# Moving the sum of the two half banks of an attention head from VectorE to ScalarE copies, transfers and GpSimd

## The chip, the cores and the metric

One core of a Trainium2 chip runs the whole kernel. The metric is the device time of one launch in microseconds (us). Engines are called by their names in the profile: PE is TensorE (PEld its weight loads), ACT is ScalarE, DVE is VectorE, POOL is GpSimd, SP is SyncE, which issues nearly all transfers.

## What is computed

A clustered attention (2 batches, 8 heads, 768 tokens, head width 64, 16 clusters per head) feeds two dense layers on 1536 tokens. Attention sees only pairs of tokens in the same cluster. The cut reference:

```python
mask = q_assign[:, :, :, None] == k_assign[:, :, None, :]
scores = scale * np.matmul(q, k.transpose(0, 1, 3, 2))
scores = np.where(mask, scores, -1000000000.0)
attn = np.exp(scores - np.max(scores, axis=-1, keepdims=True))
attn = attn / (np.sum(attn, axis=-1, keepdims=True) + 1e-09)
x = np.matmul(attn, v)                     # (B, H, S, D)
x = x.transpose(0, 2, 1, 3).reshape(B * S, H * D)
# then: h = x @ w_in; g = h * sigmoid(1.702 h); x = g @ w_out
# then: h = x @ w_in2; softmax-gated, normalised, times gains; out = ... @ w_out2
```

Matrices are split into a high part in the matmul's reduced format and a low part (the value less its high part), and products of parts are summed, so that the result keeps the accuracy of f32.

## The kernel before

**Stages.** The attention takes the first 250 us or so, the first dense layer (48 turns of weights) comes next, the second one is last.

**The attention loop.** It has 8 iterations `it` (a pair of heads, j = 0 and 1, in each) of 12 steps `n`; a step is a tile of 128 query rows, so a head has 6 steps and a half head 3. Each engine runs its own list of the same steps with lags, in the order in which the code issues them; a wait on a semaphore holds up everything behind it on its engine. In a step:

- PE: `turn` transposes the normalised rows of step n-6 (L534), then come parts of `head_half` (12 matmuls of 384 columns for a half head, spread over three steps, L551), `scores_of` (L515, L519) and, in iterations 0 to 5, one of four small pieces of the next clusters ("lots": `sims_of`, `tokens_of`, `ties_of`, `first_of` in steps 1, 4, 7, 10).
- ACT: in steps 2, 5, 8 and 11 first `x_of_low_v` (L784); then `turned_high` (two casts, L778), `exps` (L767), in steps 5 and 11 `kq_high` (L736), in steps 7 and 10 `x_high` (L790), and in steps 1 and 7 a copy for the lots (L719, L727).
- DVE: `row_max` (L958), row sums and their `inverse` (L966, L972, once for a pair of steps, two steps later), `turned_low` (two subtractions, L978), in one step of three `x_sum` (L986), and the lots' `compare` and `choose`.
- POOL: `probs` times the inverse (L1237), splits of q, k and v for the next iteration, and `x_low` (L1196) in steps 8 and 11. Its step n comes when the inverse of its pair is there, so it runs some two steps behind the others. A tiny instruction, `carry_waits` (L1161), stands ahead of several of them and takes their wait.
- SP: loads, and `place_head`, which moves parts between partitions.

**The half head's sum.** v is laid out as high beside low, so the 128 rows of a half head's bank hold the product with the high part of v in 64 rows and with the low part in the other 64; for the second head of the pair the halves are swapped. The two must be added. ACT copies the low rows of the bank to their place in `x_sums`, and DVE adds the high rows out of the bank to it:

```python
nc.scalar.copy(x_flat[D * j:D * j + D, bass.ds(x_tokens(it, n), HALF)],
               head_out(half)[D * (1 - j):D * (1 - j) + D, :]).then_inc(x_low_v_done, 1)
nc.vector.tensor_tensor(x_flat[rows, at], head_out(half)[rows, :], x_flat[rows, at], ALU.add
                        ).then_inc(x_done, 1)
```

The bank is free for PE when `x_done` has counted. With both heads of a pair summed, ACT's `x_high` casts 128 rows to `xh` and POOL's `x_low` makes `xl`, which the first dense layer reads.

Of the kernel before, what the change touches and what calls it, by code (L numbers as in the profile page):

```python
# [12 lines left out]
P = 128  # L13
# [3 lines left out]
def clustered_attention_two_mlps(nc, q_t, k_t, v_r, cent, w_gelu, w_ln, gains, out):  # L17
# [29 lines left out]
    with ExitStack() as ctx:  # L47
# [50 lines left out]
        upl = [sb(f"upl{u}", [P, DM], F32R) for u in range(2)]  # L98
        downh = [sb(f"downh{u}", [P, DM], F32R) for u in range(2)]
# [16 lines left out]
        row_inv = sb("row_inv", [P, NP], F32, early)  # L116
        probs_th = [sb(f"probs_th{h}", [P, QT, HALF], F32R, early) for h in range(2)]
# [91 lines left out]
        x_low_v_done = sem("x_low_v_done")  # L209
        x_done = sem("x_done")  # L210
# [70 lines left out]
        X_STEPS = [(c * CH + QT + CH - 1 + X_LAG + 1) % STEPS for c in range(2)]  # L281
# [5 lines left out]
        def x_tokens(it, n):  # L287

            return (it % HP) * T + (it // HP) * S + (n % QT) // CH * HALF
# [15 lines left out]
        def _(sp):  # L305
# [78 lines left out]
            for it in range(1, ITS):  # L384
# [9 lines left out]
                load_ln(it)  # L394

# [44 lines left out]
        def _(pe):  # L440
# [7 lines left out]
            def sims_of(e):  # L448
# [4 lines left out]
                if e > LOT_LEAD:  # L453
                    pe.wait_ge(x_done, (e - LOT_LEAD) * 4 - 3)
# [7 lines left out]
            def tokens_of(e):  # L462
# [3 lines left out]
                if e > LOT_LEAD:  # L466
                    pe.wait_ge(x_done, (e - LOT_LEAD) * 4 - 2)
# [6 lines left out]
            def ties_of(e):  # L474
                pe.wait_ge(compared, e + 1)
                if e > LOT_LEAD:
                    pe.wait_ge(x_done, (e - LOT_LEAD) * 4 - 1)
# [6 lines left out]
            def first_of(e):  # L484
# [3 lines left out]
                if e > LOT_LEAD:  # L488
                    pe.wait_ge(x_done, (e - LOT_LEAD) * 4)
# [223 lines left out]
        def _(act):  # L713
# [66 lines left out]

            def x_of_low_v(it, n):
                j, half = n // QT, n // CH
                act.wait_ge(head_done[j], it * 2 + half % 2 + 1)
                nc.scalar.copy(x_flat[D * j:D * j + D, bass.ds(x_tokens(it, n), HALF)],  # L784
                               head_out(half)[D * (1 - j):D * (1 - j) + D, :]).then_inc(x_low_v_done, 1)

            def x_high(it, half):

                act.wait_ge(x_done, it * 4 + 2 + half + 1)
                nc.scalar.copy(xh_flat[:, bass.ds(x_tokens(it, half * CH), HALF)],  # L790
                               x_flat[:, bass.ds(x_tokens(it, half * CH), HALF)]).then_inc(xh_done, 1)

            def attention_turn(it, steps=STEPS, last=False, drain=False):
                for n in range(steps):
                    if (exists(it, n, X_LAG - 1, STEPS) and (n - X_LAG + 1) % CH == CH - 1
                            and not (drain and n >= X_LAG - 1)):
                        x_of_low_v(*lagged(it, n, X_LAG - 1, STEPS))
# [6 lines left out]
                    if n in X_STEPS and exists(it, n, STEPS, STEPS):  # L804
                        x_high(it - 1, X_STEPS.index(n))
# [12 lines left out]
            attention_turn(ITS, X_STEPS[-1] + 1, drain=True)  # L818
# [69 lines left out]
        def _(dve):  # L888
# [93 lines left out]
            def x_sum(it, n):  # L982
                j, half = n // QT, n // CH
                dve.wait_ge(x_low_v_done, it * 4 + half + 1)
                rows, at = slice(D * j, D * j + D), bass.ds(x_tokens(it, n), HALF)
                nc.vector.tensor_tensor(x_flat[rows, at], head_out(half)[rows, :], x_flat[rows, at], ALU.add  # L986
                                        ).then_inc(x_done, 1)

            def attention_turn(it, steps=STEPS, drain=False):
                for n in range(steps):  # L990
# [6 lines left out]
                    if (exists(it, n, X_LAG, STEPS) and (n - X_LAG) % CH == CH - 1  # L997
                            and not (drain and n >= X_LAG)):
# [126 lines left out]
        def _(pool):  # L1125
# [38 lines left out]
            def scale_q(it, j):  # L1164
                pool.wait_ge(kq_loaded[j], (it + 1) * 32)
                carry_waits(STEPS + j)
# [11 lines left out]
            def v_high(it, j):  # L1178
# [4 lines left out]
                carry_waits(STEPS + 2 + j)  # L1183
# [9 lines left out]
            def x_low(it, half):  # L1193
                pool.wait_ge(xh_done, it * 2 + half + 1)
                at = bass.ds(x_tokens(it, half * CH), HALF)
# [28 lines left out]
            X_SPLIT_STEPS = [QT + 2, QT + 5]  # L1224


            def attention_turn(it, last=False):
                for n in range(STEPS):
# [18 lines left out]
                    if n in X_SPLIT_STEPS and exists(it, n, STEPS, STEPS):  # L1247
                        x_low(it - 1, X_SPLIT_STEPS.index(n))
# [71 lines left out]
```

## Time and profile before

| what | us |
|---|---|
| median of 3 runs (675.28 to 677.96) | 676.21 |
| the profiled execution's own time | 677.22 |
| its span in the trace | 675.5 |

The page gives, for the profiled execution, the busy time of each engine, the chain of work that ended last (followed back from the last instruction, at each step to what released it), and groups of instructions by line. The trace answers with rows by line, by time and by stretch. All times in it count from the span's start. A busy PE is not PE at its peak, since matmuls are pipelined.

### The profile page before, as it was taken

The numbers are of one execution on the slowest core, as the hardware profiler recorded it, in microseconds if no ns is written. First come the engines' busy times: TensorE is split into PE (matmuls) and PEld (weight loads), VectorE is DVE, ScalarE is ACT, GpSimd is POOL, SyncE is SP. The second block draws the span as 40 slices with busy tenths as digits, with TensorE's granted clock in tenths as the row PEclk, the third lists the DMA queues.
The fourth block names the chain that finished last, engine by engine and source line by source line (L and its number), as shares of the span: only waits on it lengthen the run. The fifth ranks groups of instructions, "written<-read, shape, count | busy, mean of one in ns | idle before, by whom it ended". The sixth has DMA issues, their size and how long they took to land.

```text
span 675.5 us, 10622 instructions
## 1 busy us (share of the span) xinstructions
PE 641.4 (95%) x3289; PEld 535.7 (79%) x3289; DVE 424.8 (63%) x754; ACT 323.0 (48%) x645; POOL 412.3 (61%) x586
## 2 busy tenths in 40 slices
PE   3779999999999999999999999999999999999998
PEld 1578888888888878788877888788888878888886
DVE  2678889999999985476757666662222463535352
ACT  2577888888899984222222222132222342424232
POOL 4566868787788876888878888888886100000000
PEclk9999999999999999999999999999999999999999
DMA  7665474655445330222232222222222031112101
GB/s 193 185 176 154 101 183 102 191 136 128 128 103 148 96 138 32 94 93 93 93 97 89 93 93 93 99 94 92 97 103 74 12 99 62 62 62 78 62 16 47
DMA packets 38144, 69.13 MB, mean 102 GB/s; under 512 B 4832, under 2 KB 20192, under 8 KB 38112
## 3 DMA queue, kind: packets, MB, share of 16 engines
q1 hardware_dynamic: 36384, 65.59, 33.2%
q10 hardware_dynamic: 1728, 3.15, 1.2%
q8 instruction: 16, 0.26, 0.2%
q14 instruction: 16, 0.13, 0.1%
HBM read 45.13 MB, written 3.15 MB: 71 GB/s over the span
## 4 chain that ended last, share of the span: by engine, by line
PE 74%; ACT 8%; DVE 7%; issue 5%; DMA 2%; POOL 2%; SPq 1%; POOLq 0%; DVEq 0%; ACTq 0%
PE banks L534 7%; PE banks L566 6%; PE banks L654 6%; PE banks L568 6%; PE banks L581 6%; PE banks L567 6%; PE banks L583 6%; PE banks L582 6%; PE banks L551 5%; PE banks L686 3%; PE banks L687 3%; PE banks L685 3%; ACT probs_th L778 3%; DVE probs_tl L978 3%; PE banks L657 3%
## 5 line engine op out<-in xcount | busy, mean ns | idle before, releaser
L978 DVE TENSOR_TENSOR probs_tl<-banks,probs_th 128x384 fp32r<-128x384 f32 x192 | 100.6, 548 | 20.6 <-ACT probs_th L778 19.5
L1161 POOL TENSOR_TENSOR wait_scrap<-half_power 128x1 f32<-128x1 f32 x176 | 45.7, 260 | 88.3 <-DVE row_inv L972 45.4
L778 ACT CAST probs_th<-banks 128x384 fp32r<-128x384 f32 x192 | 85.0, 483 | 30.3 <-PE banks L534 29.2
L958 DVE TENSOR_REDUCE neg_max<-banks 128x1 f32<-128x768 f32 x96 | 91.2, 950 | 13.0 <-PE banks L519 12.5
L534 PE MATMUL banks<-ident,probs 128*128 128x128 f32 x576 | 85.8, 282 | 11.8 <-DVE probs_tl L978 11.5
L767 ACT ACTIVATE probs<-banks,neg_max 128x768 f32<-128x768 f32 x96 | 87.8, 914 | 11.1 <-DVE neg_max L958 10.9
L534 PEld LDWEIGHTS banks<-ident,probs 128*128 128x128 f32 x576 | 63.9, 141 | 33.8 <-issue 25.2
L952 DVE TENSOR_TENSOR gl<-gate,gh 128x512 fp32r<-128x512 f32 x48 | 46.1, 960 | 69.6 <-ACT gh L752 69.6
L1237 POOL TENSOR_SCALAR probs<-probs,row_inv 128x768 f32<-128x768 f32 x96 | 87.0, 907 | 0.0
L1284 POOL TENSOR_TENSOR stat<-stat,half_power 128x1 f32<-128x1 f32 x12 | 6.6, 549 | 127.5 <-DVE stat L1093 127.5
L752 ACT CAST gh<-gate 128x512 fp32r<-128x512 f32 x48 | 29.8, 621 | 102.2 <-PE banks L583 57.4
L566 PE MATMUL banks<-xh,uph 128*128 (+1 forms) x192 | 76.2, 397 | 0.8 <-POOL upl L1210 0.8
L581 PE MATMUL banks<-gh,downh 128*128 128x512 f32 x192 | 76.1, 396 | 0.2
L583 PE MATMUL banks<-gh,downl 128*128 128x512 f32 x192 | 75.5, 393 | 0.0
L568 PE MATMUL banks<-xh,upl 128*128 (+1 forms) x192 | 75.4, 393 | 0.0
L567 PE MATMUL banks<-xl,uph 128*128 (+1 forms) x192 | 75.1, 391 | 0.0
L582 PE MATMUL banks<-gl,downh 128*128 128x512 f32 x192 | 74.8, 390 | 0.0
L1220 POOL TENSOR_TENSOR downl<-gelu_raw,downh 128x512 fp32r<-128x512 f32 x48 | 72.3, 1506 | 4.0
L748 ACT ACTIVATE gate<-banks 128x512 f32<-128x512 f32 x48 | 28.7, 598 | 83.4 <-PE banks L568 60.6
L551 PE MATMUL banks<-probs_th,v_parts 128*128 128x384 f32 x192 | 67.9, 353 | 0.0
L551 PE MATMUL banks<-probs_tl,v_parts 128*128 128x384 f32 x192 | 65.5, 341 | 0.0
L1210 POOL TENSOR_TENSOR upl<-gelu_raw,uph 128x512 fp32r<-128x512 f32 x48 | 62.8, 1308 | 4.0
(105 smaller groups left out, 1333.3 us busy)
## 6 DMA issues: line engine op xcount, KB each, us to landing
gelu_raw<-w_gelu SPq DMA_DIRECT2D x48, 512.0 KB, 3.3
ln_raw<-w_ln SPq DMA_DIRECT2D x8, 512.0 KB, 7.1
pair_t<-q_t SPq DMA_DIRECT2D x8, 384.0 KB, 3.5
pair_t<-k_t SPq DMA_DIRECT2D x8, 384.0 KB, 5.3
kq_raw<-k_t SPq DMA_DIRECT2D x16, 192.0 KB, 4.4
kq_raw<-q_t SPq DMA_DIRECT2D x16, 192.0 KB, 4.9
q_parts<-k_high SPq DMA_DIRECT2D x16, 192.0 KB, 2.6
q_high<-k_high SPq DMA_DIRECT2D x16, 192.0 KB, 3.0
```

The costliest lines, as they stand in the source:

```text
L534: last = nc.tensor.transpose(dst[:, t * P:(t + 1) * P], probs[:, n % NP, k * P:(k + 1) * P], ident[:])
L551: last = nc.tensor.matmul(head_out(half), v_parts[j][:, i // 2].rearrange("p two d -> p (two d)"), part[half % 2][:, i // 2, :], start=i = ...
L566: nc.tensor.matmul(hidden[u], uph[u][:, cols], xh[:, k, tok], start=k == 0, stop=False)
L567: nc.tensor.matmul(hidden[u], uph[u][:, cols], xl[:, k, tok], start=False, stop=False)
L568: last = nc.tensor.matmul(hidden[u], upl[u][:, cols], xh[:, k, tok], start=False, stop=k == KT - 1)
L581: nc.tensor.matmul(acc[d], downh[u][:, cols], gh[u][:], start=first, stop=False)
L582: nc.tensor.matmul(acc[d], downh[u][:, cols], gl[u][:], start=False, stop=False)
L583: last = nc.tensor.matmul(acc[d], downl[u][:, cols], gh[u][:], start=False, stop=end)
L767: nc.scalar.activation(probs[:, n % NP, :].rearrange("p (c t) -> p c t", c=2), scores[n % 2], ACT.Exp, bias=neg_max[:, n % NP:n % NP + 1], ...
L778: nc.scalar.copy(probs_th[half % 2][:, c * CH:(c + 1) * CH, i * P:(i + 1) * P], pt_bank(c).rearrange("p (t s) -> p t s", t=CH)).then_inc(p ...
L958: nc.vector.tensor_reduce(out=neg_max[:, col], in_=scores[n % 2], op=ALU.max, axis=mybir.AxisListType.XY, negate=True).then_inc(max_done, 1)
L978: nc.vector.tensor_tensor(probs_tl[half % 2][at], pt_bank(c).rearrange("p (t s) -> p t s", t=CH), probs_th[half % 2][at].bitcast(F32), ALU ...
```

## The change

For iterations 0 to 6 ACT copies the whole bank of a half head (128 rows) to a staging buffer, `x_parts[j][c]` (c is the half). Three transfers on SP's queue put low parts beside high ones: `x_lows[c]` gets the low rows of both heads and `x_parts[0][c]` the high rows of both. POOL then adds the two (128 rows) into `x_sums`, in its steps 9 and 11 of the next iteration. The buffers are single: ACT's copy of the next iteration waits until POOL's add of this one is done (`x_done`). PE's waits on a free bank go to `x_staged`, which ACT's copy counts. `x_high` moves to steps 1 and 3 and `x_low` to steps 3 and 5, two iterations later; the last iteration keeps the sum of before, on ACT and DVE. The carrying instructions ahead of `scale_q`, `v_high` and the pair's first `probs` go, and their waits stand on the instruction itself.

```diff
+        X_SUM_STEPS, X_HIGH_STEPS, X_LOW_STEPS = (9, 11), (1, 3), (3, 5)
+        LAST_X_STEPS = (7, 10)
...
+            def move_x(it, j, c):
+                h = it * 4 + j * 2 + c
+                low, high = slice(0, D), slice(D, P)
+                sp.wait_ge(x_staged, h + 1)
+                if j == 0:
+                    if it >= 1:
+                        sp.wait_ge(x_done, (it - 1) * 2 + c + 1)
+                    sp.dma_start(x_lows[c][low, :], x_parts[0][c][high, :]).then_inc(x_low_moved[c], 16)
+                else:
+                    sp.wait_ge(x_low_moved[c], (it + 1) * 16)
+                    sp.dma_start(x_lows[c][high, :], x_parts[1][c][low, :]).then_inc(x_parts_moved[c], 16)
+                    sp.dma_start(x_parts[0][c][high, :], x_parts[1][c][high, :]).then_inc(x_parts_moved[c], 16)
...
                 if it < ITS - 1:
                     load_kq(it + 1, 0)
+                if it >= 2:
+                    for c in range(2):
+                        move_x(it - 2, 1, c)
                 place_head(it, 1)
...
                 load_ln(it)
+                for c in range(2):
+                    move_x(it - 1, 0, c)
...
             gelu_turn(0)
+            for c in range(2):
+                move_x(ITS - 2, 1, c)
...
-                        pe.wait_ge(x_done, it * 4 + half - 1)
+                        before = it * 4 + half - 2
+                        pe.wait_ge(*((x_staged, before + 1) if before < STAGED else (x_last_done, before - STAGED + 1)))
...
+            def x_stage(it, n):
+                j, half = n // QT, n // CH
+                act.wait_ge(head_done[j], it * 2 + half % 2 + 1)
+                if it >= 1:
+                    act.wait_ge(x_done, (it - 1) * 2 + half % 2 + 1)
+                nc.scalar.copy(x_parts[j][half % 2][:], head_out(half)).then_inc(x_staged, 1)
...
-                        x_of_low_v(*lagged(it, n, X_LAG - 1, STEPS))
+                        i, m = lagged(it, n, X_LAG - 1, STEPS)
+                        (x_stage if i < ITS - 1 else x_of_low_v)(i, m)
...
-                    if n in X_STEPS and exists(it, n, STEPS, STEPS):
-                        x_high(it - 1, X_STEPS.index(n))
+                    if n in X_HIGH_STEPS and it >= 2:
+                        x_high(it - 2, X_HIGH_STEPS.index(n))
+                    if drain and n in LAST_X_STEPS:
+                        x_high(ITS - 1, LAST_X_STEPS.index(n))
...
-                    if (exists(it, n, X_LAG, STEPS) and (n - X_LAG) % CH == CH - 1
-                            and not (drain and n >= X_LAG)):
+                    if drain and (n - X_LAG) % CH == CH - 1 and n < X_LAG:
                         x_sum(*lagged(it, n, X_LAG, STEPS))
...
+            def x_sum(it, c):
+                pool.wait_ge(x_low_moved[c], (it + 1) * 16)
+                pool.wait_ge(x_parts_moved[c], (it + 1) * 32)
+                nc.gpsimd.tensor_tensor(x_flat[:, bass.ds(x_tokens(it, c), HALF)], x_parts[0][c][:], x_lows[c][:], ALU.add
+                                        ).then_inc(x_done, 1)
...
                         pool.wait_ge(inv_done, it * QT + n // 2 + 1)
-                        carry_waits(n)
...
-                    if n in X_SPLIT_STEPS and exists(it, n, STEPS, STEPS):
-                        x_low(it - 1, X_SPLIT_STEPS.index(n))
+                    if n in X_SUM_STEPS and it >= 1:
+                        x_sum(it - 1, X_SUM_STEPS.index(n))
+                    if n in X_LOW_STEPS and it >= 2:
+                        x_low(it - 2, X_LOW_STEPS.index(n))
...
                     split_up(it, r)
-                    if start and r < start + 2:
-                        x_low(ITS - 1, r - start)
+                    if start:
+                        x_low(ITS - 2, r - start)
                     split_down(*lagged(it, r, 1, RAW))
             split_turn(0, start=2)
+            for c in range(2):
+                x_low(ITS - 1, c)
```

How the order moves, in three places. First ACT in step 11 of iteration 2; before, it runs there:

```order
L790 CAST xh<-x_sums 128x384 [waits x_done]
L784 COPY x_sums<-banks 64x384 [waits head_done0]
L778 CAST probs_th0<-banks 128x3x128 [waits head_done0,turn_done0]
L778 CAST probs_th0<-banks 128x3x128 [waits turn_done1]
L767 ACTIVATE probs,row_sum<-banks,neg_max 128x768 [waits turn_done1,max_done]
L736 CAST k_high1<-kq_raw1 128x768 [waits scores_done1,q_scaled]
```

And after the change (`x_parts00` is the staging buffer of j = 0, c = 0):

```order
L821 COPY x_parts00<-banks 128x384 [waits x_done,head_done0]
L812 CAST probs_th0<-banks 128x3x128 [waits head_done0,turn_done0]
L812 CAST probs_th0<-banks 128x3x128 [waits turn_done1]
L801 ACTIVATE probs,row_sum<-banks,neg_max 128x768 [waits turn_done1,max_done]
L770 CAST k_high1<-kq_raw1 128x768 [waits scores_done1,q_scaled]
```

The cast to `xh` has left, and the copy has got a wait on `x_done`, which is now counted by POOL.

Second, POOL in steps 8 and 9 of iteration 2, before:

```order
L1161 TENSOR_TENSOR wait_scrap<-half_power 128x1 [waits inv_done]
L1237 TENSOR_SCALAR probs<-probs,row_inv 128x768
L1161 TENSOR_TENSOR wait_scrap<-half_power 128x1 [waits kq_loaded1]
L1167 TENSOR_SCALAR kq_raw1<-kq_raw1,kq_scale 128x768
L1196 TENSOR_TENSOR xl<-x_sums,xh 128x384 [waits xh_done]
L1237 TENSOR_SCALAR probs<-probs,row_inv 128x768
L1174 TENSOR_TENSOR k_low1<-kq_raw1,k_high1 128x384 [waits kq_high_done]
```

And after; the add that counts `x_done` is the fourth row:

```order
L1284 TENSOR_SCALAR probs<-probs,row_inv 128x768 [waits inv_done]
L1213 TENSOR_SCALAR kq_raw1<-kq_raw1,kq_scale 128x768 [waits kq_loaded1]
L1284 TENSOR_SCALAR probs<-probs,row_inv 128x768
L1241 TENSOR_TENSOR x_sums<-x_parts00,x_lows0 128x384 [waits x_parts_moved0,x_low_moved0]
L1220 TENSOR_TENSOR k_low1<-kq_raw1,k_high1 128x384 [waits kq_high_done]
```

The two carrying instructions are gone, `x_low` has left the pair, and the add stands at its end, behind the `probs` of step 9.

Third, ACT in steps 1 and 2 of iteration 2, before:

```order
L767 ACTIVATE probs,row_sum<-banks,neg_max 128x768 [waits turn_done1,max_done]
L719 COPY sims_t<-banks 128x384 [waits sims_done,sims_t_done]
L784 COPY x_sums<-banks 64x384 [waits head_done0]
L778 CAST probs_th1<-banks 128x3x128 [waits head_done0,turn_done0]
L778 CAST probs_th1<-banks 128x3x128 [waits turn_done1]
```

And after:

```order
L801 ACTIVATE probs,row_sum<-banks,neg_max 128x768 [waits turn_done1,max_done]
L836 CAST xh<-x_sums 128x384 [waits x_done]
L753 COPY sims_t<-banks 128x384 [waits sims_done,sims_t_done]
L821 COPY x_parts01<-banks 128x384 [waits x_done,head_done0]
L812 CAST probs_th1<-banks 128x3x128 [waits head_done0,turn_done0]
```

The cast to `xh` now stands in step 1, ahead of the lots' copy and of the next bank copy.

## Rows read from the trace of the kernel before

**Rows 1.** The page: span, busy time of each engine, chain that ended last.
```profile
span 675.5 us, 10622 instructions
...
PE 641.4 (95%) x3289; PEld 535.7 (79%) x3289; DVE 424.8 (63%) x754; ACT 323.0 (48%) x645; POOL 412.3 (61%) x586
...
PE 74%; ACT 8%; DVE 7%; issue 5%; DMA 2%; POOL 2%; SPq 1%; POOLq 0%; DVEq 0%; ACTq 0%
```

**Rows 2.** Busy time of each engine in the stretch of about one iteration.
```profile
149.00:178.40 29.40, 27.62 (x184) 24.53 (x182) 26.63 (x56) 26.01 (x58) 22.73 (x35) 1.00 0.54 143
```

**Rows 3.** Chain of waits, iteration 4: start us, us, what.
```profile
158.11 0.40 ACT xh L790
...
165.53 0.40 ACT xh L790
...
166.97 0.57 DVE probs_tl L978
...
173.63 0.26 ACT x_sums L784
```

**Rows 4.** ACT by time: start us, us, engine line, what; iterations 1, 4 to 7.
```profile
77.21 0.48 ACT L784 COPY x_sums<-banks 64x384 f32<-64x384 f32 x1
...
165.96 0.48 ACT L784 COPY x_sums<-banks 64x384 f32<-64x384 f32 x1
...
168.09 0.84 ACT L736 CAST k_high<-kq_raw 128x768 fp32r<-128x768 f32 x1
...
195.54 0.48 ACT L784 COPY x_sums<-banks 64x384 f32<-64x384 f32 x1
...
202.05 0.47 ACT L784 COPY x_sums<-banks 64x384 f32<-64x384 f32 x1
...
222.62 0.48 ACT L784 COPY x_sums<-banks 64x384 f32<-64x384 f32 x1
...
229.13 0.47 ACT L784 COPY x_sums<-banks 64x384 f32<-64x384 f32 x1
```

**Rows 5.** DVE by time, step 10 of iteration 4.
```profile
164.36 0.55 DVE L978 TENSOR_TENSOR probs_tl<-banks,probs_th 128x384 fp32r<-128x384 f32 x1
164.83 0.15 DVE L972 RECIPROCAL row_inv<-row_sum_e 128x2 f32<-128x2 f32 x1
```

**Rows 6.** POOL by time, steps 8 and 9 of iteration 4.
```profile
165.06 0.19 POOL L1161 TENSOR_TENSOR wait_scrap<-half_power 128x1 f32<-128x1 f32 x1 [0.87 <-DVE row_inv L972]
...
166.26 0.92 POOL L1167 TENSOR_SCALAR kq_raw<-kq_raw,kq_scale 128x768 f32<-128x768 f32 x1
167.14 1.00 POOL L1196 TENSOR_TENSOR xl<-x_sums,xh 128x384 fp32r<-128x384 f32 x1
168.12 0.91 POOL L1237 TENSOR_SCALAR probs<-probs,row_inv 128x768 f32<-128x768 f32 x1
169.01 1.02 POOL L1174 TENSOR_TENSOR k_low<-kq_raw,k_high 128x384 fp32r<-128x384 f32 x1
```

**Rows 7.** Groups by line: count, busy us, mean ns, idle before and its releaser.
```profile
L778 ACT CAST probs_th<-banks 128x384 fp32r<-128x384 f32 x192 | 85.0, 483 | 30.3 <-PE banks L534 29.2
...
L986 DVE TENSOR_TENSOR x_sums<-banks,x_sums 64x384 f32<-64x384 f32 x32 | 17.6, 550 | 0.5
...
L784 ACT COPY x_sums<-banks 64x384 f32<-64x384 f32 x32 | 15.1, 473 | 1.2 <-PE banks L551 0.4
```

**Rows 8.** SP by time, in step 9 of iteration 4.
```profile
162.90 0.60 SPq L324 DMA_DIRECT2D kq_raw<-q_t  x1
```

**Rows 9.** The page's transfers: issuing engine, count, KB each, us from issue to landing.
```profile
q_high<-k_high SPq DMA_DIRECT2D x16, 192.0 KB, 3.0
```

**Rows 10.** POOL by time, from attention to the first dense layer.
```profile
267.13 1.01 POOL L1196 TENSOR_TENSOR xl<-x_sums,xh 128x384 fp32r<-128x384 f32 x1 [6.19 <-ACT xh L790]
...
272.87 1.01 POOL L1196 TENSOR_TENSOR xl<-x_sums,xh 128x384 fp32r<-128x384 f32 x1
```

**Rows 11.** PE by time, in the second turn of the first dense layer.
```profile
279.58 0.50 PE L566 MATMUL banks<-xh,uph 128*128 x1 [0.80 <-POOL upl L1210]
```

More of the change, by code:

```diff
@@ L98, in clustered_attention_two_mlps @@
         upl = [sb(f"upl{u}", [P, DM], F32R) for u in range(2)]
+        stage = ExitStack()
+        x_parts = [[sb(f"x_parts{j}{c}", [P, HALF], F32, stage) for c in range(2)] for j in range(2)]
+        x_lows = [sb("x_lows0", [P, HALF], F32, stage)]
+        stage.close()
         downh = [sb(f"downh{u}", [P, DM], F32R) for u in range(2)]
@@ L209, in clustered_attention_two_mlps @@
         x_low_v_done = sem("x_low_v_done")
+        x_last_done = sem("x_last_done")
+        x_staged = sem("x_staged")
+        x_low_moved = two_sems("x_low_moved")
+        x_parts_moved = two_sems("x_parts_moved")
         x_done = sem("x_done")
@@ L279, in clustered_attention_two_mlps, with x_tokens @@
         UP_STEPS, GATE_STEPS = (2, 5), (5, 7)
-        X_STEPS = [(c * CH + QT + CH - 1 + X_LAG + 1) % STEPS for c in range(2)]
+        STAGED = 4 * (ITS - 1)
+        X_SUM_STEPS, X_HIGH_STEPS, X_LOW_STEPS = (9, 11), (1, 3), (3, 5)
+        LAST_X_STEPS = (7, 10)
         def exists(it, n, lag, per):
             return not (isinstance(it, int) and it * per + n < lag)
-        def x_tokens(it, n):
-            return (it % HP) * T + (it // HP) * S + (n % QT) // CH * HALF
+        def x_tokens(it, c):
+            return (it % HP) * T + (it // HP) * S + c * HALF
         xh_flat = xh[:].rearrange("p k t -> p (k t)")
@@ L453, in sims_of @@
                 if e > LOT_LEAD:
-                    pe.wait_ge(x_done, (e - LOT_LEAD) * 4 - 3)
+                    pe.wait_ge(x_staged, (e - LOT_LEAD) * 4 - 3)
                 for x in range(2):
@@ L783, in x_of_low_v, with x_high @@
                 act.wait_ge(head_done[j], it * 2 + half % 2 + 1)
-                nc.scalar.copy(x_flat[D * j:D * j + D, bass.ds(x_tokens(it, n), HALF)],
+                nc.scalar.copy(x_flat[D * j:D * j + D, bass.ds(x_tokens(it, half % 2), HALF)],
                                head_out(half)[D * (1 - j):D * (1 - j) + D, :]).then_inc(x_low_v_done, 1)
[L787 to L791, printed above, removed]
+            def x_high(it, c):
+                if it < ITS - 1:
+                    act.wait_ge(x_done, it * 2 + c + 1)
+                else:
+                    act.wait_ge(x_last_done, 2 + c + 1)
+                at = bass.ds(x_tokens(it, c), HALF)
+                nc.scalar.copy(xh_flat[:, at], x_flat[:, at]).then_inc(xh_done, 1)
             def attention_turn(it, steps=STEPS, last=False, drain=False):
@@ L983, in x_sum @@
                 j, half = n // QT, n // CH
-                dve.wait_ge(x_low_v_done, it * 4 + half + 1)
-                rows, at = slice(D * j, D * j + D), bass.ds(x_tokens(it, n), HALF)
+                dve.wait_ge(x_low_v_done, half + 1)
+                rows, at = slice(D * j, D * j + D), bass.ds(x_tokens(it, half % 2), HALF)
                 nc.vector.tensor_tensor(x_flat[rows, at], head_out(half)[rows, :], x_flat[rows, at], ALU.add
-                                        ).then_inc(x_done, 1)
+                                        ).then_inc(x_last_done, 1)
             def attention_turn(it, steps=STEPS, drain=False):
@@ L1190, in v_low, with x_low @@
                                         ALU.subtract).then_inc(v_low_done, 1)
-            def x_low(it, half):
-                pool.wait_ge(xh_done, it * 2 + half + 1)
-                at = bass.ds(x_tokens(it, half * CH), HALF)
+            def x_sum(it, c):
[3 more added lines that the diff above has]
+                                        ).then_inc(x_done, 1)
+            def x_low(it, c):
+                pool.wait_ge(xh_done, it * 2 + c + 1)
+                at = bass.ds(x_tokens(it, c), HALF)
                 nc.gpsimd.tensor_tensor(xl_flat[:, at], x_flat[:, at], xh_bits_flat[:, at], ALU.subtract
@@ L1251, in attention_turn @@
                     if last and n == STEPS - 1:
+                        pool.wait_ge(x_done, 2 * (ITS - 1))
                         split_down(0, 0)
```

12 lines of the change are left out of this document (5 added, 7 removed).

## Prediction

> **What bounds the kernel now.** I read the page first [rows 1]: PE is busy for 95% of the span and holds 74% of the chain that ended last; ACT, DVE and POOL share most of the rest. That says where the launch as a whole is limited, not what this change is worth, since it touches the attention loop alone. There the stretch of one iteration [rows 2] shows four engines at 22.7 to 27.6 us of 29.4, none of them full. Such a picture means a cycle of waits through several engines, so the next view is the chain in order of time.
>
> In the loop the bank copies of step 11 start at 77.21 in iteration 1, 165.96 in iteration 4, 195.54 in iteration 5 and 222.62 in iteration 6 [rows 4]: 29.58 us an iteration while the lots run, 27.08 in iteration 6, which has none. In the chain of iteration 4 the same round comes four times, once for three steps: PE from one `turn` to the next, ACT from that `turn`'s cast through an `exp` and everything that stands behind it (cast to `xh` 0.40 us, bank copy, first cast of the next step), then one `turned_low` on DVE, 0.57, which lets PE go on [rows 3]. In one round of the four DVE takes ACT's place, with the lots' comparison. Two things follow. The adds on DVE that the change takes away (28 of the 32, 0.55 us each [rows 7]) stand in none of these rounds: VectorE does them while the chain is on PE or ACT. And whatever is put before ACT's casts in the steps with a bank copy lengthens a round in full, since the next `turn` waits for that cast.
>
> **The change part by part.** *What leaves DVE* I cost at nothing: 28 adds, 15.4 us busy, all beside the chain. One small effect is kept: in step 10 of iteration 4 the first `turned_low` starts at 164.36 and the inverse at 164.83 [rows 5]; with an add less ahead of it DVE is there when ACT's cast is ready, about 0.17 earlier.
>
> *ACT's copy* handles 128 rows instead of 64 with the same 384 columns. The old one takes 0.473 us [rows 7], and I take 0.48, at no cost.
>
> *The wait in step 11.* This is the term that decides. The staging buffer of half c = 0 is filled by ACT in step 11 of iteration `it`, and must have been read by POOL's add of iteration `it` - 1, which POOL does at the end of its step 9 of the same `it`. POOL runs late by design: its step 8 waits for the inverse of rows 8 and 9, which DVE makes in step 10. From the rows of iteration 4: the inverse starts 0.17 earlier than 164.83, at 164.66, and ends 0.15 later, at 164.81 [rows 5]. POOL begins 0.08 after an inverse (165.06 after 164.98 [rows 5, 6]), so at 164.89. It then has `probs` of row 8, `scale_q`, `probs` of row 9 (0.89, 0.88 and 0.89, from start to start [rows 6]) and the add, for which the nearest row is `x_low`, the same shape on the same engine, 1.00 [rows 6]: 164.89 + 2.66 + 1.00 = 168.55. With 0.05 for the signal ACT's copy starts at 168.60 where it started at 165.96 [rows 4], 2.64 us later. ACT can do nothing else meanwhile: casts, `exp` and `kq_high` of step 11 are queued behind the copy, DVE's `turned_low` behind the cast, PE's next `turn` behind that. As the copy was on the chain, the shift is not made up later. It comes in iterations 1 to 6 (iteration 0 has no predecessor, 7 uses the old path): 6 × 2.64 = 15.8 us.
>
> The removed carrying instructions (0.16 each, from 165.06 to the next start) are already counted as gone in this sum; if the wait costs as much on the instruction itself, 0.16 × 6 = 1.0 comes on top.
>
> *The same wait in step 2.* The half c = 1 is staged in step 2 and needs POOL's add of step 11. After the late copy, `k_high` ends 168.09 + 0.84 - 165.96 = 2.97 later [rows 4]; POOL then has two `k_low` (1.01), two `probs` and the add: 2.97 + 0.1 + 2.02 + 1.77 + 1.0 = 7.86. With lots ACT comes to that copy 173.63 - 165.96 = 7.67 after the one in step 11 [rows 3, 4], plus 0.40 for the cast that now stands in step 1: 8.07, so no wait. Into iterations 6 and 7 the distance is 202.05 - 195.54 = 6.51 and 229.13 - 222.62 = 6.51 [rows 4], with the cast 6.91: a wait of 0.95 and the cast of 0.40, of which PE may hide some 0.1. I take 1.2 twice, 2.4 us, bounds 0 and 2.7.
>
> *The casts to `xh`.* Each is 0.40 on the chain, in steps 7 and 10 [rows 3]. The one in step 7 goes in iterations 1 to 7, -2.8; the one in step 10 lies ahead of the new wait, so it pays only in iteration 7, -0.4; the new one in step 1 stands before the lots' copy in iterations 2 to 5, +1.6 (6 and 7 are counted above). The one in step 3 falls where ACT waits for PE. Sum -1.6.
>
> *POOL's load.* In an iteration it gets two adds, +2.0, and loses ten carrying instructions, -1.6; it is busy for 22.7 of 29.4 [rows 2] and stays off the chain but for its place ahead of ACT.
>
> *SP and the transfers.* The four moves that the add needs are queued behind `kq_raw`, whose last issue ends at 163.50 [rows 8], 0.55 to 0.6 each: the two for c = 0 go out by 164.7. The nearest row, twice the bytes between the same partitions, lands 3.0 after its issue starts [rows 9]: by 167.1, and the add comes at 167.55. I cost this at nothing, though the margin is 0.4; landing 1 us later would cost 0.6 × 6 = 3.6. Behind the moves waits `place_head` of the second head, which needs `k_high` (start 168.09) anyway, while the moves are out by 165.9.
>
> *Into the first dense layer.* POOL's 6.19 us of waiting for the last cast goes, since `x_low` of iteration 6 stands there [rows 10]. But its own next step waits for PE, and then both `x_low` of iteration 7 stand ahead of the split that PE is already waiting for (0.80 idle before 279.58 [rows 11]), where one stood before (272.87 [rows 10]). Up to 1.0 later, 0 if the DVE leaves POOL alone; I take +0.4.
>
> Sum: 15.8 + 2.4 - 1.6 + 0.4 = +17.0 us. Against the profiled execution's 677.2 (span 675.5 and 1.7 around it) that is 694.2; the median of the runs is 1.0 lower, so 693.2 us.
>
> **A rule against the change.** What the rows show is an add of 384 columns on POOL in 1.00 us [rows 6] beside 0.55 on DVE [rows 7]. The Trainium skill (GPSIMD Engine Reference, section 4.1, Engine selection) says to leave elementwise adds to VectorE, since GpSimd takes about twice as long with two inputs. The rows agree with it on the ratio. By that rule the only price is the slower adder, and it is a rival below; the trace prices the place of the add in the order as well.
>
> **The rivals.**
> *The wait is half paid by waits that exist.* ACT idles 29.2 us behind PE in the loop [rows 7], some 3 an iteration; if half of the shift is made up there, the first term is 7.9, and the time 685.3. For it: no engine is full. Against it: those idle times end on PE, which waits for ACT's own cast, so the late copy shifts them too. Chance 0.12.
> *The add is in time.* Then the sum without its two waits: -1.6 + 0.4 + 0.8 for two casts, about -0.4: 675.8, no change. It needs POOL 2.6 us earlier, before the inverse exists. Chance 0.05.
> *Only the slower adder counts.* 1.00 - 0.55 on the chain six times, 2.7: 678.9, within 0.5%. It would need the three instructions ahead of the add to be done when ACT arrives. Chance 0.04.
> *DVE is the bound after all.* If each of the 28 adds lay on a round, the loop would lose about 0.5 × 28 = 14 us, and even with one or two of the waits the time is about 664. It decides if the chain's rounds pass through DVE's adds; the chain shows none. Chance 0.05.
>
> **How the numbers follow.** The forecast, 693.2, has 0.74. Its own bounds: carrying price +1.0, late transfers +3.6, step 2 from -2.4 to +0.3, dense layer from -0.4 to +0.6: 690 to 699. The range goes down to the half paid wait with a little room, 684 to 699; below it lie the in-time, slower-adder and DVE cases, 0.14. 0.5% (3.4 us) is about what a measurement of this kernel can tell from no change. Faster by more 0.05, within it 0.09, slower by more 0.86.
>
> **What would show it.** In the profile after, ACT's bank copies should have an idle time behind POOL's add, six of some 2.6 to 3.3 us and two near 1; the copies of step 11 should lie 32.2 us apart in iterations 2 to 5. DVE should be busy some 15 us less, POOL much the same. The forecast is wrong if ACT's copies wait for PE alone, or if the copies stand 29.6 apart with the waits in place, or if POOL's adds wait for the transfers.

## The result, and the profile after

The changed kernel takes 702.18 us (median of 4 runs, 700.32 to 702.53) against 676.87 before (4 runs): a ratio of 1.037, 95% interval 1.034 to 1.040. The forecast, 693.2, had the sign and the place; the time lies above its range, and 25.3 us were added where 17.0 were forecast. The profiled execution has a span of 700.6, against 675.5 in [rows 1].

The page of the kernel after: span, busy time, and the chain that ended last.

```profile
span 700.6 us, 10635 instructions
...
PE 647.2 (92%) x3289; PEld 543.3 (78%) x3289; DVE 412.6 (59%) x726; ACT 318.1 (45%) x645; POOL 412.9 (59%) x520
...
PE 70%; DMA 7%; DVE 5%; POOL 5%; ACT 4%; SPq 4%; issue 4%; ACTq 0%; POOLq 0%; DVEq 0%
```

Beside [rows 1], DVE is busy 12.2 us less (some 15 were forecast) and POOL the same. But PE is busy 5.8 us longer with the same 3289 matmuls, and DMA and SP's queue, 3% of the chain before, now hold 11%. The forecast had no term for the first; the second it put at nothing, with a bound of 3.6.

One row of the waits in the attention loop (who waited for whom: us in total, times, longest):

```profile
ACT x_parts L821 <- POOL x_sums L1241: 26.2, 7, 6.6
```

That is the forecast's wait. ACT by time shows the seven of them, six in step 11 and one in step 2 (start, duration, line, operation; in brackets the idle time before):

```profile
77.59 0.48 ACT L821 COPY x_parts<-banks 128x384 f32<-128x384 f32 x1 [4.88 <-POOL x_sums L1241]
112.20 0.48 ACT L821 COPY x_parts<-banks 128x384 f32<-128x384 f32 x1 [3.55 <-POOL x_sums L1241]
147.25 0.48 ACT L821 COPY x_parts<-banks 128x384 f32<-128x384 f32 x1 [6.60 <-POOL x_sums L1241]
180.91 0.48 ACT L821 COPY x_parts<-banks 128x384 f32<-128x384 f32 x1 [3.32 <-POOL x_sums L1241]
214.41 0.48 ACT L821 COPY x_parts<-banks 128x384 f32<-128x384 f32 x1 [3.53 <-POOL x_sums L1241]
245.41 0.48 ACT L821 COPY x_parts<-banks 128x384 f32<-128x384 f32 x1 [3.20 <-POOL x_sums L1241]
253.25 0.48 ACT L821 COPY x_parts<-banks 128x384 f32<-128x384 f32 x1 [1.08 <-POOL x_sums L1241]
```

The copies of step 11 answer to [rows 4]. They lie 34.61, 35.05, 33.66, 33.50 and 31.00 us apart, where it was 29.58 four times and 27.08 once. The forecast had 32.2. From the first to the last of them that is 167.82 against 145.41: +22.4. The first stands 0.4 later than before, and from the last to the end of the span it is 455.2 instead of 452.9, +2.3. Together +25.1, the difference of the spans.

The waits differ, so something besides POOL's order sets them. POOL's adds by time, with what they waited for themselves:

```profile
76.51 0.99 POOL L1241 TENSOR_TENSOR x_sums<-x_parts,x_lows 128x384 f32<-128x384 f32 x1 [1.63 <-DMA x_parts<-x_parts]
111.12 0.99 POOL L1241 TENSOR_TENSOR x_sums<-x_parts,x_lows 128x384 f32<-128x384 f32 x1 [0.32 <-DMA x_parts<-x_parts]
146.17 0.99 POOL L1241 TENSOR_TENSOR x_sums<-x_parts,x_lows 128x384 f32<-128x384 f32 x1 [3.37 <-DMA x_parts<-x_parts]
179.84 0.99 POOL L1241 TENSOR_TENSOR x_sums<-x_parts,x_lows 128x384 f32<-128x384 f32 x1
213.34 0.99 POOL L1241 TENSOR_TENSOR x_sums<-x_parts,x_lows 128x384 f32<-128x384 f32 x1 [0.29 <-DMA x_parts<-x_parts]
244.34 0.99 POOL L1241 TENSOR_TENSOR x_sums<-x_parts,x_lows 128x384 f32<-128x384 f32 x1
```

Four of the six waited for their transfers, two of them long. And the waits alone don't explain the distances: 34.61 ends with a wait of 3.55, 33.50 with one of 3.53. The 8 us behind each late copy (the stretch and its length, the busy time and instructions of PE, PEld, DVE, ACT and POOL, then the granted clock of PE, DMA share, GB/s; 1.00 is full clock, 2.4 GHz, and 0.50 half, 1.2 GHz, so a value between them is a mean over the stretch):

```profile
77.59:85.59 8.00, 6.40 (x30) 4.78 (x30) 3.99 (x8) 4.59 (x11) 4.72 (x5) 0.57 0.36 76
112.20:120.20 8.00, 6.40 (x46) 5.43 (x47) 5.81 (x12) 7.12 (x17) 4.75 (x5) 1.00 0.36 75
147.25:155.25 8.00, 6.40 (x33) 5.37 (x34) 4.19 (x9) 5.23 (x12) 4.73 (x5) 0.63 0.36 75
180.91:188.91 8.00, 6.40 (x35) 4.66 (x36) 4.46 (x10) 5.58 (x13) 4.73 (x5) 0.79 0.36 75
214.41:222.41 8.00, 6.40 (x27) 6.33 (x28) 4.81 (x10) 5.76 (x13) 4.73 (x5) 0.57 0.36 75
245.41:253.41 8.00, 6.40 (x42) 5.92 (x42) 5.85 (x12) 6.90 (x16) 4.77 (x5) 1.00 0.36 74
```

Behind four of the six stalls PE runs a part of this stretch at half clock: it is busy for 6.40 us each time, but gets 46 matmuls done at a clock of 1.00 and 30 at 0.57. In the iteration of the kernel before that [rows 2] shows it is 1.00 throughout. So there are three candidates for what the forecast left out: the moves, the clock, and something at the end. The experiments take them one by one.

### The profile page after: what moved, and what is told of

Same layout as the page of the kernel before. It is cut to its first block, busy times and chain, and to the rows that moved or that the text cites. A ratio compares the mean times of both kernels' runs of the same rounds, so it can differ in the third digit from the quotient of the medians.

```text
span 700.6 us, 10635 instructions
## 1 busy us (share of the span) xinstructions
PE 647.2 (92%) x3289; PEld 543.3 (78%) x3289; DVE 412.6 (59%) x726; ACT 318.1 (45%) x645; POOL 412.9 (59%) x520
## 4 chain that ended last, share of the span: by engine, by line
PE 70%; DMA 7%; DVE 5%; POOL 5%; ACT 4%; SPq 4%; issue 4%; ACTq 0%; POOLq 0%; DVEq 0%
PE banks L600 6%; PE banks L602 6%; PE banks L601 6%; PE banks L615 6%; PE banks L688 6%; PE banks L617 6%; PE banks L616 6%; PE banks L567 5%; PE banks L585 5%; PE banks L720 3%; PE banks L721 3%; PE banks L719 3%; DMA q_high<-k_high 3%; PE banks L691 3%; PE banks L548 2%
## 5 line engine op out<-in xcount | busy, mean ns | idle before, releaser
L567 PEld LDWEIGHTS banks<-ident,probs 128*128 128x128 f32 x576 | 66.9, 144 | 50.1 <-issue 37.6
L585 PE MATMUL banks<-probs_tl,v_parts 128*128 128x384 f32 x192 | 67.3, 350 | 0.0
L548 PE MATMUL banks<-k_high,q_parts 128*128 128x384 f32 x192 | 56.9, 379 | 7.5 <-DMA k_low<-hot_t 6.3
```

Source lines behind the costliest of these rows:

```text
L567: last = nc.tensor.transpose(dst[:, t * P:(t + 1) * P], probs[:, n % NP, k * P:(k + 1) * P], ident[:])
L585: last = nc.tensor.matmul(head_out(half), v_parts[j][:, i // 2].rearrange("p two d -> p (two d)"), part[half % 2][:, i // 2, :], start=i = ...
```

## The experiments

**The moves earlier (moves_early, moves_first).** Two ways of giving POOL's add its data in time, with the add left where it is.

```
--- moves_early, SP (the loop, iteration it)
 load_kq(it, 1)
+if it >= 2: move_x(it - 2, 1, 0)
 place_head(it, 0); load_v(it, 0); load_kq(it + 1, 0)
-for c in range(2): move_x(it - 2, 1, c)
+move_x(it - 2, 1, 1)
--- moves_first, SP
 place_head(it, 0)
+for c in range(2): move_x(it - 2, 1, c)
 load_v(it, 0); load_kq(it + 1, 0)
-for c in range(2): move_x(it - 2, 1, c)
```

> The changed kernel, with the two moves of half c = 0 (second head) issued ahead of the first head's placing instead of behind the loads, some 8 us earlier; POOL's order is untouched. In the changed kernel ACT's seven waits for POOL's add sum to 26.2 us, four of those adds themselves wait for a transfer (1.63, 0.32, 3.37 and 0.29 us). Theory (late transfers are the part of the wait that the forecast left out): no add waits for a transfer any more, the six waits of step 11 become about 3.3 each, and the time falls by 5 to 6 us, to some 696.5. Rival (the adds are late because POOL is late, and the transfers' share is only a wait that overlaps it): the waits stay and the time is 701 to 703.

> The changed kernel, with the moves of the second head's parts still behind the first head's placing on SP, but ahead of the value and the q and k loads (three issues, 1.6 us) instead of behind them. Theory (the moves are late because of the loads just ahead of them, by their issue and by sharing the transfer engines): no add waits for a transfer, ACT's waits of step 11 are 3.2 to 3.5 each, as with the early moves, and the time is 695 to 698. Rival (the placing ahead of them is late itself, held by its own transfers): the small waits go, the large one (6.60 us) falls by some 1.6 us only and stays above 4.5, the time 699 to 701.

Measured: 696.82 us (690.34 to 699.48) and 697.78 (693.98 to 698.82). In both no add waits for a transfer, and every wait of step 11 is 3.20 to 3.22. The theory's times came in both: by the medians late moves cost 5.4 us by the one and 4.4 by the other, with several us between executions of one kernel. The rival of moves_first (a large wait above 4.5 remains) fell: to be ahead of the value, q and k loads was enough.

**The weight loads as the cause (ln_later).** The 512 KB weight loads of iterations 1 to 4 were moved to iterations 5 and 6, and those of 5 and 6 to 7.

```
--- ln_later, SP
-load_ln(it)
+for u in {5: (1, 2), 6: (3, 4), 7: (5, 6, 7)}.get(it, ()):
+    load_ln(u)
```

> The changed kernel, with the 512 KB weight loads of iterations 1 to 4 issued in iterations 5 to 7 instead; moves and POOL's order untouched. Theory (the moves are late because the heads' own moves ahead of them in SP's queue land late, behind loads that fill the transfer engines): the two large waits of ACT, 4.88 and 6.60 us, shrink to some 3.3, and the time to 697. Rival (the loads have no part, SP's order alone delays the moves): the waits stay as they were and the time within 2 us of 702.

Measured: 701.28 us. The waits changed (3.33, 3.46, 5.12, 3.50, 4.83, 3.21), but four adds still waited for their moves, and the time is the rival's. The large waits shrank and the fifth grew, in the iteration to which loads were moved; so the weight loads have a part, but they aren't what makes the moves late. In iteration 3 of the changed kernel SP's order shows where the time goes (start, duration, line):

```profile
130.68 0.60 SPq L354 DMA_DIRECT2D q_high<-k_high  x1
...
136.51 0.46 SPq L354 DMA_DIRECT2D k_high<-k_high  x1
...
142.88 0.60 SPq L389 DMA_DIRECT2D x_parts<-x_parts  x1
```

`k_high` waits for `q_high` to land, which took some 5.8 us there; all that follows in SP's queue, the move for the add last, is late with it, and lands shortly before the add at 146.17. What made that transfer slow stays open.

**The clock (filler, moves_filler).** 24 small matmuls into columns that nothing reads, where PE stands still; once in the changed kernel, once with the early moves, so that every stall has the same length.

```
--- filler and moves_filler, PE (attention_turn)
 for n in range(steps):
+    if n == 1 and not drain and it >= 2:
+        for _ in range(24):
+            nc.tensor.matmul(banks[:, 7, HALF:HALF + P], first_w[:], first_w[:], start=False, stop=False)
```

> The changed kernel with 24 extra small matmuls on PE, into columns that nothing reads, in the place where PE stands still while ACT waits (step 1, iterations 2 to 7). Theory (the stall costs twice: its own length, and then a spell of half clock in which five head matmuls take 1.60 us instead of 0.87): the clock stays at full rate behind the stalls and the time falls by 4 to 7 us, to 695 to 698, with ACT's waits as they were. Rival (the spell of half clock is hidden, since ACT sets the pace there): within 1.5 us of 702. If the extra matmuls outlast the stall, the time rises instead.

> The kernel with the early moves, and the 24 extra small matmuls on PE where it stands still in step 1 of iterations 2 to 7. With the early moves every wait of step 11 is 3.2 us, so the extra matmuls (2.8 us together) should fill most of PE's idle time each time. In the kernel with the early moves the copies of step 11 lie 33.20, 33.21 and 34.26 us apart. Theory (the spell of half clock behind the stall costs on top of the wait): with the clock kept, they lie 32.0 to 32.3 apart, ACT's waits stay at 3.2, and the time is 6 to 10 us less than with the early moves alone, some 689. Rival (half clock is hidden): the copies stay 33.2 apart and the time within 2 us of 697.

The first is inconclusive: 701.27 us (696.53 to 704.19). The moves are late there as in the changed kernel, ACT's waits are 27.4 in all, and two spells of half clock stayed. The second tells more, since its waits of step 11 are all 3.21 or 3.22. The 8 us behind its copies of step 11:

```profile
76.53:84.53 8.00, 8.00 (x63) 7.01 (x62) 5.80 (x12) 7.11 (x17) 4.74 (x5) 1.00 0.47 103
108.22:116.22 8.00, 7.64 (x58) 6.52 (x57) 5.78 (x11) 7.09 (x17) 4.76 (x5) 1.00 0.37 77
139.89:147.89 8.00, 8.00 (x38) 8.00 (x37) 2.93 (x7) 4.20 (x9) 1.26 (x2) 0.52 0.50 119
177.69:185.69 8.00, 8.00 (x62) 7.00 (x62) 5.80 (x12) 7.11 (x17) 4.76 (x5) 1.00 0.45 97
209.38:217.38 8.00, 7.62 (x53) 6.96 (x52) 5.85 (x12) 6.91 (x16) 4.76 (x5) 1.00 0.36 75
239.30:247.30 8.00, 7.64 (x54) 7.03 (x52) 5.85 (x12) 6.90 (x16) 4.77 (x5) 1.00 0.36 74
```

Each row begins at a copy, so the starts give the distances: 31.69, 31.67, 37.80, 31.69, 29.92. Three of the first four, with the clock at 1.00, are 1.5 to 2.6 us shorter than the 33.20, 33.21 and 34.30 in their places in moves_early, where it was 0.79, 0.79 and 0.57. The last is 29.95 in moves_early, with 1.00 there too. One went wrong: PE had idled 1.69 us for a placed row just before, the extra matmuls ran at half clock, and outlasted the stall:

```profile
140.47 5.22 PE L646 MATMUL banks<-first_w 128*128 128x128 f32 x24
```

In the profiled execution that one cost 6.1 us (37.80 against 31.69). The time, 693.51 us (691.81 to 696.38), is 3.3 lower than that of moves_early instead of the 6 to 10 expected, and the two ranges overlap; it is the distances that show the price.

The cleanest price stands in moves_first, where no matmuls were added. The same view:

```profile
78.50:86.50 8.00, 6.41 (x35) 5.03 (x36) 4.47 (x10) 5.60 (x13) 4.73 (x5) 0.79 0.37 77
111.72:119.72 8.00, 6.41 (x46) 5.43 (x47) 5.81 (x12) 7.12 (x17) 4.76 (x5) 1.00 0.36 76
143.42:151.42 8.00, 6.40 (x35) 5.09 (x36) 4.48 (x10) 5.60 (x13) 4.73 (x5) 0.79 0.59 144
176.64:184.64 8.00, 6.40 (x46) 5.42 (x47) 5.78 (x11) 7.10 (x17) 4.77 (x5) 1.00 0.36 74
208.34:216.34 8.00, 6.40 (x34) 6.21 (x35) 5.17 (x11) 6.49 (x15) 4.74 (x5) 0.79 0.48 116
238.56:246.56 8.00, 6.40 (x33) 6.21 (x34) 5.23 (x11) 6.65 (x15) 4.74 (x5) 0.79 0.36 75
```

The first four distances are 33.22, 31.70, 33.22, 31.70: with a spell of 0.79 behind the stall 33.22, with 1.00 31.70, and PE's stall is the same in both (the rows behind the first two copies, PE by time):

```profile
80.09 0.92 PE L567 MATMUL banks<-ident,probs 128*128 128x128 f32 x6 [2.98 <-DVE probs_tl L1026]
...
113.31 0.92 PE L567 MATMUL banks<-ident,probs 128*128 128x128 f32 x6 [2.98 <-DVE probs_tl L1026]
```

So in an iteration with lots a spell costs 1.52 us at 0.79, and 2.6 at 0.57 (34.30 in moves_early against 31.70). Without lots it costs less: the fifth distance, 30.22 at 0.79, is 0.3 longer than the 29.92 of moves_filler at 1.00, and ACT's wait of 1.07 in the next step 2, which moves_filler has, is absent there. That the stall brings the spell on is shown by moves_filler, where PE was kept busy in it and the clock behind stayed at 1.00 in five of six; why one stall of 2.98 us does and the next doesn't is open. The Trainium skill (TensorE: Matmul & The Clock Gate, HAM oscillation — how this bites in real kernels) tells of the same pattern: a loop in which PE idles in each turn goes back to half rate in each turn and pays for it beside the idle time. The rows agree in part: behind six stalls of 2.98 to 3.00 us in moves_first the clock fell four times, not each time.

**The add's place (sum_early, sum_early2).** The early moves, and POOL's add of half c = 0 in step 6 instead of 9; in sum_early2 one more move is issued earlier.

```
--- sum_early = moves_early and
-X_SUM_STEPS, X_HIGH_STEPS, X_LOW_STEPS = (9, 11), (1, 3), (3, 5)
+X_SUM_STEPS, X_HIGH_STEPS, X_LOW_STEPS = (6, 11), (1, 3), (3, 5)
--- sum_early2 = sum_early and, SP
 place_head(it, 1)
+move_x(it - 1, 0, 0)
 load_v(it, 1); load_pair(it + 3); load_ln(it)
-for c in range(2): move_x(it - 1, 0, c)
+move_x(it - 1, 0, 1)
```

> The kernel with the early moves, and POOL's add of half c = 0 in step 6 instead of step 9, so ahead of the inverse of rows 8 and 9. Theory (the place of the add in POOL's order is the cost): ACT's copy of step 11 waits for PE only, the 25.1 us of waits in step 11 go, the spells of half clock behind them go with them (about 1.5 us each in four iterations), and with 702.2 as the start the time is 669 to 674, below the kernel before. Rival 1 (the add in step 6 makes POOL's rows late, and PE waits for them instead): 680 to 690. Rival 2 (VectorE's relief and the moved casts are worth nothing): no better than the kernel before, 676 to 678.

> The kernel with early moves and the add in step 6, and the first head's move of half c = 0 also issued earlier, ahead of the value, pair and weight loads. In the kernel without that, this move took 8.68 us to land behind those loads, and SP waited for it ahead of the first head's placing. Theory (the chain there goes through SP and its moves now): the placing is no longer held up, the waits of PE for the placed rows (4.4 us in the loop) go, and the time is 668 to 672. Rival (the placing has slack, the loop's pace is set by ACT, DVE and PE): 673 to 676.

Measured: 674.43 us (671.38 to 677.17, 10 runs; ratio to the kernel before 0.9974, interval 0.9952 to 0.9997) and 676.64 (671.64 to 680.34, 10 runs; 1.0009, 0.9978 to 1.0040). ACT by time in sum_early, step 11 of iterations 1 to 3:

```profile
75.85 0.49 ACT L822 COPY x_parts<-banks 128x384 f32<-128x384 f32 x1
...
104.63 0.49 ACT L822 COPY x_parts<-banks 128x384 f32<-128x384 f32 x1
...
133.77 0.49 ACT L822 COPY x_parts<-banks 128x384 f32<-128x384 f32 x1
```

No wait is left in step 11, and the clock behind all six copies is 1.00. The five distances are 28.78, 29.14, 28.76, 30.20 and 26.93, and 22.4 us are back beside 696.82 with the moves alone (with the spells of half clock behind the stalls). The time is 0.4 above the theory's range and below both rivals'. That settles the main cause: not POOL's speed, but that in step 9 the add stands behind an inverse and three more instructions that aren't done when ACT arrives. In sum_early2 the distances are 28.79, 28.79, 28.81, 28.92 and 26.95, in all 1.6 us less than in sum_early, and PE's waits for placed rows between 60 and 235 us fall from 1.9 to 0.2. So in the profiled executions the placing was on the path for 1.6 us. Yet the median is no better, 0.6 above the rival's range, and the mean granted clock was lower (0.989 to 0.997 over its ten runs, 0.994 to 1.000 in sum_early). The 668 to 672 of the theory fell; what the earlier move is worth stays open.

**The end (after_spread, sum_spread, sum_spread2).** In the changed kernel two low parts on POOL stand ahead of a split for which PE waits in the dense layer (POOL, then PE, by time):

```profile
297.92 2.36 POOL L1247 TENSOR_TENSOR xl<-x_sums,xh 128x384 fp32r<-128x384 f32 x2
...
303.09 0.62 PE L600 MATMUL banks<-xh,uph 128*128 x1 [2.19 <-POOL upl L1261]
```

The wait was 0.80 before [rows 11]; now it is 2.19, and the matmuls behind it run at half clock. These kernels put the two behind later splits.

```
--- after_spread = the changed kernel and, POOL; sum_spread = sum_early and the same
 split_up(it, r)
+if it == 1 and r >= 2: x_low(ITS - 1, r - 2)
 ...
 split_turn(0, start=2)
-for c in range(2): x_low(ITS - 1, c)
+split_turn(1)
--- sum_spread2 = sum_spread, X_SUM_STEPS = (6, 9), move_x(it - 2, 1, 1) right behind place_head(it, 0)
```

> The changed kernel; only POOL's two low parts of iteration 7, which stand in a row ahead of the first split that PE waits for in the dense layer, are put behind the third and fourth split of the next turn, one each. From the copy of step 11 in iteration 6 to the end of the span the kernel before takes 452.9 us and the changed one 455.2. Theory (the two in a row make PE wait, and a spell of half clock follows): this stretch shrinks to 451 to 453, the time to 698 to 700. Rival (PE's wait there is hidden): unchanged, 455 and 702.

> The kernel with early moves and the add in step 6, with the same spreading of the two low parts. In the kernel without the spreading the copies of step 11 lie 28.8 to 29.1 us apart (29.58 before the change), and PE waits for POOL's split in the first dense layer. Theory (what was gained in the loop is given back there): the time falls by 2 to 4 us, to 670.5 to 672.5, clear of the kernel before. Rival: 674 to 676 as without it.

> As the last, with the add of half c = 1 in step 9 instead of 11, and its move ahead of the value load, so that ACT's two remaining waits of 1.07 us in step 2 of iterations 6 and 7 go. Theory: some 1 to 2 us less than the last, 669 to 671. Rival (the add in step 9 now waits for its transfer and makes the rows behind it late): no gain, or up to 1 us an iteration more, 672 to 678.

Measured: after_spread 700.10 us (697.97 to 700.67). From the copy of step 11 in iteration 6 (243.63) to the end of the span (696.3) it takes 452.7 instead of 455.2, and PE no longer waits there: the term is 2.5 us by the trace, 2.1 by the medians. sum_spread takes 673.07 (9 runs), 0.9945 of the kernel before, interval 0.9922 to 0.9968; sum_spread2 672.99, 0.9938 (0.9912 to 0.9965), which can't be told apart. In sum_spread2 the two waits of 1.07 are gone, but four adds wait for their transfers instead (5.3 us in all), as its rival had it, so what the two waits cost stays open. Both kernels are some 0.6% faster than the kernel before. The 670.5 to 672.5 expected of sum_spread was slightly too low: against sum_early 1.4 us came by the medians and 2.0 by the ratios, where 2 to 4 were expected.

**What the change takes away (before_no_carry, before_tiny_sum).** The kernel before without the carrying instructions of the loop, and the kernel before with 28 of VectorE's adds cut to one column.

```
--- before_no_carry, POOL: in scale_q, v_high and attention_turn
-carry_waits(...)
--- before_tiny_sum, DVE: x_sum
+if it < ITS - 1: at = bass.ds(x_tokens(it, n), 1)
-head_out(half)[rows, :]
+head_out(half)[rows, 0:1 if it < ITS - 1 else HALF]
```

> The kernel before, with only the carrying instructions of the attention loop taken out (norm, scale, value copy), as the change does. Theory (they lie beside the chain in the loop): only the one in the first scale at the start shows, 0.8 us, so 676. Rival (POOL sits on the chain in the loop): 88 instructions of 0.20 us, up to 10 us less, 666 to 671.

> The kernel before, with 28 of VectorE's 32 adds cut to one column, so their work is left out and only their place in the queue is kept. Theory (the adds lie beside the chain): 675 to 677. Rival (each add delays the next subtraction by its length): 28 x 0.45 = 12.6 us less, some 663; half of it would be 670.

Measured: 676.15 us, a ratio of 1.0004 (0.9981 to 1.0026), and 674.84, 0.9972 (0.9951 to 0.9993). The adds in the second one (both forms):

```profile
L988 DVE TENSOR_TENSOR x_sums<-banks,x_sums 64x1 f32<-64x1 f32 (+1 forms) x32 | 6.4, 200 | 0.5
```

11 us of VectorE's work are gone (17.6 in [rows 7]), and 1.5 off the time. So nearly all of the adds' time was beside the chain. The carrying instructions bring nothing that can be told from none.

## Why the prediction was off, point by point

The five distances of step 11, split by what the experiments priced: 2.12 for the wait at full clock with the data in time (31.70 less 29.58), four times, and 2.84 in the last (29.92 in moves_filler less 27.08), 11.3 us; late moves, the waits above 3.20, 0.35 + 3.40 + 0.12 + 0.33 = 4.2; what is left, 2.56, -0.05, 1.84, 1.47 and 1.08, is 6.9 and goes with the clock in the rows behind each copy (0.57, 1.00, 0.63, 0.79, 0.57). Sum 22.4. With the first copy (its wait of 4.88, 1.7 of it late moves, less a start 4.5 earlier) and 2.3 at the end that is the 25.1 of the spans.

- **The wait in step 11: right in place and kind, near in size.** It was forecast at 2.64; it measures 2.12 against the kernel before and 2.9 against the same kernel without it (31.70 less 28.79). The loop without the wait runs 0.8 us shorter than before; the casts explain 0.4 of that by the forecast's own terms and VectorE's adds some 0.1 (29.48 in before_tiny_sum); the rest wasn't split.
- **"The shift is not made up later": right, but not the whole price.** This is the step that failed first: a stall of a few us that ACT hands on to PE was costed as a delay, with nothing for what PE does afterwards. Behind it PE ran at half clock for some us in most iterations: 6.9 us in the loop, with no term and no bound in the forecast. The chain of the kernel before had PE as the longest part of the round, 3.10 us of the 7.04 from 160.63 to 167.67, so any slowing of PE there had to count in full:

```profile
160.63 0.98 PE banks L534 x6
161.61 0.35 PE banks L515 x2
161.96 0.35 PE banks L519 x2
162.31 0.88 PE banks L551 x5
163.19 0.17 PE banks L490
163.36 0.37 PE banks L534 x3
```

  The trace of the kernel before held a hint as well. In the loop's first iteration PE idles once for 3.53 us, and the clock over 47 to 52 us is 0.66 (the stretch is shown below, with the start). From 62 to 245 us PE never idles for 0.7 us at a time in that kernel:

```profile
46.53 0.62 PE L515 MATMUL banks<-k_high,q_parts 128*128 128x384 f32 x2 [3.53 <-DMA k_low<-hot_t]
```

- **"I cost this at nothing, though the margin is 0.4": wrong, and the bound was too small.** Six delays of 1 us were allowed; in fact two were large (1.63 and 3.37) and two small, because the placing ahead of the moves can itself be held. Late moves cost 4.4 to 5.4 us by the two experiments. The queue's issue times were read from one iteration; the landing times of what it waits for were not.
- **The step-2 wait.** Forecast at two of about 1: the copy at 253.25 has one of 1.08. The other is absent because PE's half clock had already made ACT late in iteration 6; without that (moves_filler) both are there, 1.07 each. In moves_early, with 1.00 in iteration 6 and 0.57 in 7, only the first is.
- **Into the first dense layer.** +0.4, bounds -0.4 to +0.6 around it: it measures 2.3 against the kernel before and 2.5 against after_spread, with the spell of half clock. The two low parts in a row took 2.36, which the rows of before (1.0 each) did tell.
- **Against all that, the start.** ACT was ready for its copy in iteration 1 at 72.71 (77.59 less 4.88), 4.5 before the 77.21 of [rows 4]. The casts of steps 7 and 10 are 0.8 of that, and 0.4 wasn't split. Some 1.0 is there at the first bank copy (41.38 against 42.42): POOL's first scaling starts 0.77 earlier, though the carrying instruction ahead of it takes up 0.17 only; in the kernels without that instruction it starts anywhere from 7.52 to 8.79, with the landing of the first loads. Another 2.3 lie between the first copy and the second, where PE waits for placed rows and the kernel before then has a spell of half clock that the kernel after hasn't. It is there in all three profiled kernels without the change (0.66 to 0.81 from 47 to 52 us) and varies between those with it (0.50 to 1.00), so most of the 4.5 is luck of the profiled executions as far as is known. The stretch in the kernel before, then after:

```profile
47.00:52.00 5.00, 5.00 (x25) 4.66 (x27) 3.62 (x7) 1.85 (x4) 2.11 (x4) 0.66 0.65 176
```

```profile
47.00:52.00 5.00, 5.00 (x38) 4.09 (x37) 3.25 (x8) 3.59 (x9) 2.75 (x3) 1.00 0.56 127
```

- **The rivals.** The wait half paid by idle time that exists: fell, 2.9 of 3.2 us are paid. The add in time: its time, 675.8, is what sum_early measures (674.43), so that sum came close, some of it by an earlier start (the first copy at 75.85 against 77.21); the changed kernel just isn't that case. DVE as the bound: fell, by before_tiny_sum. Only the slower adder: fell. The Trainium skill (GPSIMD Engine Reference, section 4.1, Engine selection) has the add take about twice as long on GpSimd, and the trace agrees for 384 columns (1.0 against 0.55). Here one add on POOL, with 128 rows, stands for two on DVE, with 64, and in sum_early the same adds on the same engine cost nothing that shows.

## What to carry to other kernels

When a step is moved to an engine that runs late by design, ask first what stands ahead of it there and who can't start without it; here three steps of order were worth some 22 us, and the engine's speed nothing that shows. A stall that ends on TensorE can have a second price behind it, the time at half clock (6.9 us in this loop): take it as a bound wherever a forecast adds stalls of some us to a loop in which TensorE was never idle that long, and give the data of a cross-engine hand-over more margin than one iteration's issue times suggest.

## What the runs showed of the hardware that was not expected

Two stalls of PE of the same 2.98 us, an iteration apart in one execution, were followed by a granted clock of 0.79 and of 1.00 over the next 8 us, and by iterations of 33.22 and 31.70 us. A transfer between partitions that landed in some 3 us at one time took 5.8 at another in the same loop, and in sum_early one move behind pair and weight loads took 8.68.
